# One pair of heads per step, the last query rows of both heads in one tile, and high q doubled by transfers within SBUF

## The chip, the core and the metric

The kernel runs on one core of one Trainium2 chip. A core has TensorE (PE; its weight loads are listed as PEld), VectorE (DVE), ScalarE (ACT), GpSimd (POOL) and SyncE (SP), which here only issues DMAs. They share SBUF (128 partitions), PE writes into PSUM, and 16 DMA engines move data. The time is the device's, in microseconds (us), and lower is better.

## The reference

Three stages run one after the other; the change is in the first alone.

```python
# attention, 4 x 8 heads, S = 576, D = 64
scores = q @ k.T / 8                     # per head
bias   = -(cum[:, None] - cum[None, :])  # cum = cumsum(max(s, 0))
scores = where(causal, -1e9, scores + minimum(bias, 0))
attn   = exp(scores - rowmax); attn /= attn.sum(-1) + 1e-9
x      = attn @ v                        # heads side by side: 576 x 512 per batch
# then: gated MLP with a product over tokens (moe), then 8 experts, one per token (moe2)
```

## The kernel before, in words

A program is written out per engine; engines meet only at semaphores, and each runs its instructions in the order in which they are written. 32 heads make 16 pairs. A head has 576 query rows: four tiles of 128 and a last one of 64 (`rows_of`); tile i needs the keys up to 128(i+1).

The precision scheme: q and k are split into a high and a low part. `q1` holds high q in a head's own 64 partitions and low q in the other 64, `k1` holds high k in both halves, `k2` low k beside four rows of the bias ("aug"), `q2` high q beside its four rows. So a tile of scores is two matmuls (`q1`·`k1`, L786, and `q2`·`k2`, L788) and one that adds the causal mask (L793). The second place of high q and of high k is filled by GpSimd's copies (`twice`, L484 and L487 for the main 512 columns, L476 and L477 for the last 64).

The loop runs over single heads, t = 0 to 33 (L862 on PE). Step t makes the scores of head t, DVE takes the row maxima (`row_max`, L661), ACT the exponentials with their sums (`exps`, L551), and PE turns the probabilities of head t-1 in four groups (`turn_probs`, L806) through the two banks of `tbank`; DVE (L667) and ACT (L558) copy each group out. The five tiles of scores share four banks of `sbank`: the last tile takes the place of tiles 0 and 1. In every second step the pair's k and q are turned (L748, L765, L755) through `obank`, the sums are inverted, widened on GpSimd (L495) and turned (L812), and the product with v of a finished pair (`attend`, L837, two parts) is written to `obank` and scaled by DVE into `xT` (L688).

SyncE issues, per pair, four DMAs of the bias rows (L398, L399), eight for k and q (L391 with 128 KB, L393 with 16 KB) and four for v (L405, L407), each group behind one semaphore wait. Ahead of the loop it issues the first loads, stores the bias rows to DRAM and reads them back (L420 to L399), and loads the MLP's weights (L425, L426). All of these go to one DMA queue. GpSimd splits the MLP's weights in 16 shares beside the loop (`weights`).

Of the kernel before, what the change touches and what calls it, by code (L numbers as in the profile page):

```python
# [13 lines left out]
P = 128  # L14
# [3 lines left out]
def moe_block(nc, q, k, v, s, w_in, g_ln, w_sg, b_sg, w_out, w_gate, w_local, w1, w2, out):  # L18
# [21 lines left out]
    PT_COLS = sum((i + 1) * w for i, w in enumerate([P] * FULL + [LAST]))  # L40
# [9 lines left out]
    aug_dram = nc.dram_tensor("aug_dram", (HEADS, 2, 4, S), F32).ap()  # L50
# [3 lines left out]
    with stack:  # L54
# [3 lines left out]
        def tensors(scope):  # L58
# [58 lines left out]
        recip_wide = ab("recip_wide", [P, ST, 2, D], F32)  # L117
        recipT = ab("recipT", [P, S], F32)
        probs = [ab(f"probs{u}", [P, OFF_P[-1] + SP], F32) for u in range(2)]
        k_raw = [ab(f"k_raw{u}", [P, ST, 2, D], F32) for u in range(2)]  # L120
        q_raw = [ab(f"q_raw{u}", [P, ST, 2, D], F32) for u in range(2)]
# [5 lines left out]
        nmax = [ab(f"nmax{u}", [P, ST], F32) for u in range(2)]  # L127
        sums = [ab(f"sums{u}", [P, 2, ST], F32) for u in range(2)]
        sums_eps = ab("sums_eps", [P, 2, ST], F32)
        recip = ab("recip", [P, 2, ST], F32)  # L130
# [101 lines left out]
        late_pads = sem("late_pads")  # L232
# [9 lines left out]
        aug_in = [sem(f"aug_in{c}") for c in range(4)]  # L242
        v_in = [sem(f"v_in{u}") for u in range(2)]
        kq_turned = sem("kq_turned")
        kq_high = sem("kq_high")
        kq_low = sem("kq_low")
        kq_twice = sem("kq_twice")
        scored = sem("scored")
        maxed = sem("maxed")
        exped = sem("exped")  # L250
        p_turned = sem("p_turned")
        p_left = [sem(f"p_left{n}") for n in range(4)]
# [3 lines left out]
        recip_turned = sem("recip_turned")  # L256
        recip_main = sem("recip_main")
# [65 lines left out]
        MAIN, TAIL = slice(0, FULL * P), slice(FULL * P, S)  # L323
        SHARES = 16
        FIRST_SHARE = 4
        own_rows = [slice(0, D), slice(D, P)]
        other_rows = [slice(D, P), slice(0, D)]
        wide_of = [sbank[:, 2 * i:2 * i + 2, :].rearrange("p a n -> p (a n)") for i in range(2)]

        GROUPS_OF = [[(0, 0), (0, 1), (0, 2)],  # L330
                     [(1, 1), (1, 2), (2, 2)],
                     [(0, 3), (0, 4), (1, 3), (1, 4)],
                     [(2, 3), (2, 4), (3, 3), (3, 4), (4, 4)]]
        GROUP_COLS = [sum(rows_of[i] for _, i in g) for g in GROUPS_OF]
        GROUP_AT = [sum(GROUP_COLS[:n]) for n in range(4)]
        ROWS = [slice(0, 3 * P), slice(3 * P, S)]
        R_TAIL = slice(3 * P, 3 * P + LAST)
        K_TAIL, Q_TAIL = slice(0, LAST), slice(LAST, 2 * LAST)

        def score_view(i, rows):  # L340
            if i < FULL:
                return sbank[0:rows, i, 0:W_P[i]]
            return sbank[0:rows, 0:2, 0:HALF]

        def probs_view(u, i, rows):
            w = probs[u][0:rows, OFF_P[i]:OFF_P[i] + W_P[i]]
            return w if i < FULL else w.rearrange("p (a n) -> p a n", a=2)
# [12 lines left out]
        def sets_of(p):  # L360
            return [2 * (p % 2), 2 * (p % 2) + 1]

        def k_pair(t):

            return (t + 3) // 2 if t % 2 and (t + 3) // 2 < PAIRS else None

        def q_pair(t):

            return t // 2 + 1 if t % 2 == 0 and t // 2 + 1 < PAIRS else None

        def inverted_pair(t):

            return t // 2 - 1 if t % 2 == 0 and t >= 2 else None

        def attended_pair(t):

            return t // 2 - 1 if t % 2 and t >= 3 else None

# [6 lines left out]
        def _(sp):  # L385
            def load_kq(p):
                b = p % 2
                for u in range(2):
                    for raw, src in ((k_raw, kf), (q_raw, qf)):
                        x = src[2 * p + u, :, :]  # L390
                        sp.dma_start(raw[b][:, 0:FULL, u, :],  # L391
                                     x[0:FULL * P, :].rearrange("(t p) d -> p t d", p=P)).then_inc(kq_in[b], 16)
                        sp.dma_start(raw[b][0:LAST, FULL, u, :], x[FULL * P:S, :]).then_inc(kq_in[b], 16)  # L393

            def load_aug(h):
                c = h % 4
                r = 0 if h % 2 else D
                sp.dma_start(k2[c][r:r + 4, :].bitcast(F32), aug_dram[h, 0, :, :]).then_inc(aug_in[c], 16)  # L398
                sp.dma_start(q2[c][r:r + 4, 0:S].bitcast(F32), aug_dram[h, 1, :, :]).then_inc(aug_in[c], 16)  # L399

            def load_v(p):
                b = p % 2
                for u in range(2):
                    x = vf[2 * p + u, :, :]
                    sp.dma_start(v_raw[b][:, 0:FULL, u, :],  # L405
                                 x[0:FULL * P, :].rearrange("(t p) d -> p t d", p=P)).then_inc(v_in[b], 16)
                    sp.dma_start(v_raw[b][0:LAST, FULL, u, :], x[FULL * P:S, :]).then_inc(v_in[b], 16)  # L407
# [12 lines left out]
            sp.dma_start(aug_dram, aug[:, :, :, :]).then_inc(aug_stored, 16)  # L420
            sp.wait_ge(aug_stored, 16)
            sp.wait_ge(consts, 2)
            load_aug(0)
            load_aug(1)
            sp.dma_start(win_raw[:, :, :], w_in.rearrange("(k p) n -> p k n", p=P)).then_inc(w_in_landed, 16)  # L425
            sp.dma_start(wout_raw[:, :, :], w_out.rearrange("(k p) n -> p k n", p=P)).then_inc(w_out_landed, 16)  # L426
            sp.wait_ge(late_sets, 6)
            load_aug(2)
            load_aug(3)
            load_v(0)  # L430
            load_v(1)
            for t in range(2, HEADS):
                if t + 2 < HEADS:
                    sp.wait_ge(scored, ST * (t - 1))
                    load_aug(t + 2)
                m = t // 2
                if t % 2 == 0 and m + 1 < PAIRS:
                    sp.wait_ge(kq_turned, 3 * m)
                    load_kq(m + 1)
                if t % 2 == 0 and m >= 2:  # L440
                    sp.wait_ge(av_done[1], m - 1)
                    load_v(m)

        @block.gpsimd
        def _(pool):
# [12 lines left out]
            pool.wait_ge(pool_own, 6)  # L458
            for u in range(2):
                nc.gpsimd.memset(v_raw[u][:, FULL, :, :], 0.0)  # L460
                nc.gpsimd.memset(q1[2 + u][:, S:SP].bitcast(F32), 0.0).then_inc(late_sets, 1)
            for u in range(2):
                pool.wait_ge(late_sets, 2 + u)
                nc.gpsimd.memset(k2[2 + u][other_rows[u], :].bitcast(F32), 0.0)
                nc.gpsimd.memset(q2[2 + u][other_rows[u], :].bitcast(F32), 0.0).then_inc(late_sets, 1)
            pool.wait_ge(late_sets, 4)
            for u in range(2):
                nc.gpsimd.memset(q2[2 + u][own_rows[u], S:SP].bitcast(F32), 0.0).then_inc(late_sets, 1)
                pool.wait_ge(late_sets, 5 + u)

            def twice(p, n):

                if n == 4:
                    pool.wait_ge(kq_high, 5 * p + 5)
                    for u, c in enumerate(sets_of(p)):
                        nc.gpsimd.tensor_copy(k1[c][other_rows[u], TAIL], k1[c][own_rows[u], TAIL].bitcast(F32))  # L476
# [14 lines left out]
            def widen(m):  # L491
                pool.wait_ge(inverted, m + 1)
                if m:
                    pool.wait_ge(recip_turned, m)
# [1311 lines left out]
```

## Time and profile before

| what | value |
|---|---|
| median of 3 runs | 879.79 us (879.1 to 881.36) |
| the profiled execution | 881.97 us, span 880.2 us |
| busy over the span | PE 775.4 us (88%), DVE 486.0, ACT 378.7, POOL 163.6 |
| chain that ended last | PE 82%, DVE 10%, ACT 3% |
| attention's scores begin, xT is whole | 28.06 us, 283.7 us |

The profile is of one execution. A busy PE row counts a matmul from its start to a modelled end, so neighbours overlap; where the pace matters, the distance between starts is read. "Idle before" is what an engine waited ahead of a group, and the name behind the arrow is what released it.

### The profile page before, as it was taken

Reading aid. Unit: us, or ns where it says so; the run is one execution under the profiler, and the core shown is the slowest. Engines: PE = TensorE matmul, PEld = TensorE weight load, DVE = VectorE, ACT = ScalarE, POOL = GpSimd, SP = SyncE. Lnnn points to the kernel's source line nnn. Section 1 sums busy time; section 2 is a strip of 40 time slices with the busy share of each in tenths; the row PEclk is TensorE's granted clock in tenths of the full one; section 3 lists DMA queues with packets and bytes.
Section 4 is the critical chain, followed back from the end, with each engine's and each line's share of the span. In section 5 each row is a group of like instructions: output and inputs, shape, how many; then the busy total and the mean of one; then the engine's idle time right before and its main releaser. Section 6 shows DMA issues by size and latency. Waiting matters only on the chain.

```text
span 880.2 us, 15547 instructions
## 1 busy us (share of the span) xinstructions
PE 775.4 (88%) x4885; PEld 649.7 (74%) x4886; DVE 486.0 (55%) x947; ACT 378.7 (43%) x846; POOL 163.6 (19%) x341
## 2 busy tenths in 40 slices
PE   2778888788888999999999997579999999999993
PEld 2566667566676899989899895458888888887772
DVE  8577777877775363453462353854644663726221
ACT  2576676766765340431431512334442551533110
POOL 4134454532222100000000000021122122221121
PEclk9999999999999999999999998579999999999997
DMA  6622232222210000010010012961543561611110
GB/s 156 192 57 57 58 71 54 54 64 57 64 26 23 3 1 1 1 54 0 0 54 0 0 55 71 365 239 38 222 164 119 206 235 49 225 32 34 41 42 16
DMA packets 81405, 70.41 MB, mean 80 GB/s; under 512 B 61960, under 2 KB 61960, under 8 KB 81322
## 3 DMA queue, kind: packets, MB, share of 16 engines
q1 hardware_dynamic: 77354, 58.49, 21.6%
q0 software_dynamic: 4000, 11.28, 3.9%
q8 instruction: 27, 0.44, 0.2%
q14 instruction: 24, 0.20, 0.1%
HBM read 59.72 MB, written 11.86 MB: 81 GB/s over the span
## 4 chain that ended last, share of the span: by engine, by line
PE 82%; DVE 10%; ACT 3%; issue 2%; DMA 1%; SPq 0%; POOL 0%; POOLq 0%; ACTq 0%; DVEq 0%
PE sbank L1091 25%; PE sbank L1684 10%; PE sbank L1686 9%; PE sbank L1685 9%; PE obank L837 5%; PE tbank L806 5%; PE sbank L786 4%; DVE nmax L661 3%; PE sbank L788 3%; PE obank L1139 2%; ACT probs L551 1%; DVE q L653 1%; PE tbank L1669 1%; PE tbank L1709 1%; PE sbank L793 1%
## 5 line engine op out<-in xcount | busy, mean ns | idle before, releaser
L551 ACT ACTIVATE probs<-sbank,nmax 128x128 f32<-128x128 f32 (+4 forms) x160 | 90.6, 568 | 62.3 <-DVE nmax L661 60.8
L806 PE MATMUL tbank<-ident,probs 128*128 128x128 f32 x480 | 75.7, 279 | 20.5 <-ACT pT L558 20.1
L786 PE MATMUL sbank<-k,q 128*128 128x256 f32 (+2 forms) x192 | 74.4, 393 | 16.3 <-ACT probs L551 14.7
L661 DVE TENSOR_REDUCE nmax<-sbank 128x1 f32<-128x128 f32 (+4 forms) x160 | 80.1, 532 | 7.5 <-PE sbank L793 5.9
L1684 PE MATMUL sbank<-w_high,xsT_h 128*128 x184 | 75.0, 407 | 1.9 <-DVE xsT_l L1609 1.7
L1193 DVE TENSOR_TENSOR w_low<-w_low,w_high (+1 forms) x64 | 74.0, 1218 | 0.7 <-ACT w_high L1549 0.3
L1686 PE MATMUL sbank<-w_low,xsT_h 128*128 x184 | 72.7, 395 | 0.0
L1685 PE MATMUL sbank<-w_high,xsT_l 128*128 x184 | 72.5, 394 | 0.0
L1684 PE MATMUL sbank<-w_high,hidT_h 128*128 x176 | 71.0, 403 | 0.1
L806 PEld LDWEIGHTS tbank<-ident,probs 128*128 128x128 f32 x480 | 51.1, 141 | 25.7 <-ACT pT L558 23.9
L1549 ACT CAST w_high<-w_low (+1 forms) x64 | 62.3, 1053 | 17.5 <-SPq L1438 17.5
L1686 PE MATMUL sbank<-w_low,hidT_h 128*128 x176 | 68.9, 391 | 0.0
L1685 PE MATMUL sbank<-w_high,hidT_l 128*128 x176 | 68.8, 391 | 0.0
L1480 POOL DMA_INDIRECT out_dram<-y,sid x25 | 25.3, 1011 | 217.8 <-DVE y L1645 214.4
L1469 POOL COPY gid<-slots 128x1 int32 (+1 forms) x25 | 6.4, 255 | 290.1 <-DVE slots L1369 281.5
L788 PE MATMUL sbank<-k,q 128*128 128x256 f32 (+2 forms) x192 | 60.3, 319 | 0.0
L786 PEld LDWEIGHTS sbank<-k,q 128*128 128x128 f32 x192 | 37.9, 197 | 23.5 <-ACT probs L551 18.3
L1572 ACT CAST hidT_h<-tbank 128x512 fp32r<-128x512 f32 x22 | 12.9, 586 | 92.8 <-PE tbank L1709 92.8
L1645 DVE TENSOR_SCALAR y<-sbank,sid 128x512 f32<-128x512 f32 x22 | 16.5, 751 | 64.1 <-PE sbank L1686 63.3
L837 PE MATMUL obank<-pT,v_raw 128*64 128x192 f32 (+4 forms) x512 | 50.2, 339 | 0.3 <-ACT recipT L562 0.3
L1091 PE MATMUL sbank<-wsg_h,vn_h 128*128 128x288 f32 x160 | 48.3, 302 | 2.2 <-DVE vn_l L1025 1.9
L1091 PE MATMUL sbank<-wsg_l,vn_h 128*128 128x288 f32 x160 | 47.9, 299 | 0.0
(246 smaller groups left out, 1939.7 us busy)
## 6 DMA issues: line engine op xcount, KB each, us to landing
w_low<-in_moe_w_dram SPq DMA_DIRECT2D x16, 2048.0 KB, 14.1
k_raw<-in_k_dram SPq DMA_DIRECT2D x32, 128.0 KB, 2.3
q_raw<-in_q_dram SPq DMA_DIRECT2D x32, 128.0 KB, 2.4
v_raw<-in_v_dram SPq DMA_DIRECT2D x32, 128.0 KB, 2.3
x_dram<-x SPq DMA_DIRECT2D x4, 1024.0 KB, 4.4
win_raw<-in_moe_w_in_dram SPq DMA_DIRECT2D x1, 2048.0 KB, 7.9
wsg_raw<-in_moe_w_sg_dram SPq DMA_DIRECT2D x1, 1152.0 KB, 5.8
wout_raw<-in_moe_w_out_dram SPq DMA_DIRECT2D x1, 1024.0 KB, 10.8
```

The lines of the kernel that those rows point to most:

```text
L551: nc.scalar.activation(probs_view(u, i, r), score_view(i, r), ACT.Exp, bias=nmax[u][0:r, i:i + 1], accum_out=sums[(t // 2) % 2][0:r, u, i: ...
L661: nc.vector.tensor_reduce(nmax[u][0:r, i:i + 1], score_view(i, r), ax, ALU.max, negate=True).then_inc(maxed, 1)
L786: nc.tensor.matmul(dst, q1[c][:, q_cols], k1[c][:, cols], start=True, stop=False)
L788: nc.tensor.matmul(dst, q2[c][:, q_cols], k2[c][:, cols], start=False, stop=last)
L806: mm = nc.tensor.transpose(tbank[:, n % 2, at:at + P], probs[h % 2][:, OFF_P[i] + P * j:OFF_P[i] + P * (j + 1)], ident[:, :])
L837: mm = nc.tensor.matmul(obank[own_rows[u], c, lo:lo + w], v_raw[m % 2][:, j, u, :], pT[(2 * m + u) % 3][:, at:at + w], start=(j == 0), sto ...
L1091: mm = nc.tensor.matmul(dst, a[:, i, lhs_cols], b[:, i, rhs_cols], start=(n == 0), stop=(n == 3 * len(pairs) - 1))
L1193: nc.vector.tensor_sub(w, w.bitcast(F32), piece(w_high, high_place, i).bitcast(F32)).then_inc(wlow_done, 1)
L1549: nc.scalar.copy(piece(w_high, high_place, i), piece(w_low, low_place, i).bitcast(F32)).then_inc(whigh_done, 1)
L1684: nc.tensor.matmul(dst, xh, wh, start=first, stop=False)
L1685: nc.tensor.matmul(dst, xl, wh, start=False, stop=False)
L1686: return nc.tensor.matmul(dst, xh, wl, start=False, stop=last)
```

## The change

Attention alone is rewritten; all that stands behind it is the same code.

- The loop runs over pairs, g = 0 to 18. In step g PE turns q and k of pair g, makes all scores of pair g-1 but tile 3 of its second head, finishes pair g-2 (that tile, the rest of the turned probabilities, the second part of the product with v, the sums) and makes the first part of the product with v of pair g-3.
- The last 64 query rows of both heads stand in one 128-row tile: `q1` and `q2` of the second head hold their columns shifted by 64 with zeros beside them, so that four pairs of matmuls add up in two banks (`last_scores`); one maximum and one exponential serve both heads, and its four key blocks are turned into one bank and kept in `pT4`. The second part of the product with v has separate matmuls for these 64 columns.
- k, q and their last rows are copied out of PSUM in one instruction of 128 partitions (before: one per head), high q into the new tile `q_both`. Four transfers within SBUF per pair, 64 x 576 fp32 each (147 KB), bring it from there into `q1` and `q2` of both heads (`double_q`). GpSimd copies k only.
- SyncE's loads of the last rows of two heads are one DMA; its order per pair is bias rows, `double_q`, k and q of the next pair, the last bias row, v.

```diff
@@ SyncE
+            def load_aug(m):
+                c, b = sets(m), m % 2
+                sp.dma_start(k2[c + 1][AUG_ROWS[1], :].bitcast(F32), aug_k_dram[2 * m + 1, :, :]).then_inc(aug_in[b], 16)
+                for u in range(2):
+                    sp.dma_start(q2[c + u][AUG_ROWS[u], Q_ALL[u]].bitcast(F32),
+                                 aug_q_dram[2 * m + u, :, BOTH_ALL[u]]).then_inc(aug_in[b], 16)
+            def double_q(m):
+                sp.wait_ge(tails_high, m + 1)
+                for u in range(2):
+                    for t in (q1, q2):
+                        sp.dma_start(t[sets(m) + u][OWN[u], Q_ALL[u]].bitcast(F32),
+                                     q_flat[OWN[u], BOTH_ALL[u]].bitcast(F32)).then_inc(q_doubled[m % 2], 16)
...
-            for t in range(2, HEADS):
-                if t + 2 < HEADS:
-                    sp.wait_ge(scored, ST * (t - 1))
-                    load_aug(t + 2)
...
+            for m in range(1, PAIRS):
+                if m >= 2:
+                    sp.wait_ge(scored[1][3], m - 1)
+                load_aug(m)
+                double_q(m)
+                if m + 1 < PAIRS and m >= 1:
+                    sp.wait_ge(k_turned, m)
+                    load_kq(m + 1)
+                sp.wait_ge(k2_copied, m + 1)
+                load_aug_k(m)
+                if m >= 2:
+                    sp.wait_ge(av_done[0], m - 1)
+                load_v(m)
@@ ScalarE: q leaves PSUM once the copies of the pair before have read q_both
+            def split_q(m):
+                act.wait_ge(q_turned, m + 1)
+                if m:
+                    act.wait_ge(q_doubled[(m - 1) % 2], 64 * turn_of(m - 1))
+                nc.scalar.mul(q_flat[:, BOTH_MAIN], obank[:, 1, :], SCALE).then_inc(q_high, 1)
@@ TensorE
+            def last_scores(m):
+                for a in range(2):
+                    for u in range(2):
+                        score(sbank[:, a, 0:HALF], sets(m) + u, Q_LAST[u], slice(a * HALF, (a + 1) * HALF),
+                              u == 0, u == 1 and a == 0)
+                nc.tensor.matmul(sbank[:, 1, HALF - LAST:HALF], ident_bf[:, :], mask_last[:, :], start=False,
+                                 stop=True).then_inc(last_scored, 1)
...
+            for g in range(PAIRS + 3):
+                a, b, c = g - 1, g - 2, g - 3
+                if alive(g):
+                    turn_q(g)
+                if alive(b):
+                    pe.wait_ge(exped[0][3], b + 1)
+                    scores(1, 3, b)
+                if alive(c):
+                    pe.wait_ge(recip_main, c + 1)
+                    pe.wait_ge(left[1][0], c + 1)
+                    attend(c, 0)
...
+                if alive(a):
+                    pe.wait_ge(q_doubled[a % 2], 64 * turn_of(a))
+                    pe.wait_ge(k1_copied, 3 * a + 3)
+                    pe.wait_ge(aug_in[a % 2], 48 * turn_of(a))
+                    pe.wait_ge(aug_k_in[a % 2], 16 * turn_of(a))
+                    scores(0, 0, a)
+                    scores(0, 1, a)
```

On PE, in the middle of the stage, the rows from one pair's first part of the product with v to the next tiles of scores. Before (`pT` is a turned probability tile, `probs` one not yet turned, `k1_1` the set 1 of `k1`):

```order
L806 MATMUL tbank<-ident,probs0 128x128 x2
L837 MATMUL obank<-pT0,v_raw1 64x384 [waits recip_main,v_in1,recip_tail,p_left1,p_left0]
L837 MATMUL obank<-pT1,v_raw1 64x384
L837 MATMUL obank<-pT0,v_raw1 64x256
L837 MATMUL obank<-pT1,v_raw1 64x256
L837 MATMUL obank<-pT0,v_raw1 64x128
L837 MATMUL obank<-pT1,v_raw1 64x128
L786 MATMUL sbank<-k1_1,q1_1 128x384
```

And now:

```order
L763 MATMUL obank<-ident,q_raw0 128x128 [waits x_left1,kq_in0]
L763 MATMUL obank<-ident,q_raw0 128x128 x3
L792 MATMUL sbank<-k1_1,q1_1 128x512 [waits exped03]
L793 MATMUL sbank<-k2_1,q2_1 128x512
L800 MATMUL sbank<-mask_bf,ident_bf 128x128
L839 MATMUL obank<-pT0,v_raw1 64x384 [waits left10,recip_main]
L839 MATMUL obank<-pT1,v_raw1 64x384
L839 MATMUL obank<-pT0,v_raw1 64x256
L839 MATMUL obank<-pT1,v_raw1 64x256
L839 MATMUL obank<-pT0,v_raw1 64x128
L839 MATMUL obank<-pT1,v_raw1 64x128
```

The turning of q with its wait for the loads (`kq_in0`) now stands ahead of the product, three instruction groups apart, at the head of the step.

On SP, one pair of the loop before:

```order
L398 DMA k2_0<-aug_dram 4x576 [waits scored]
L399 DMA q2_0<-aug_dram 4x576
L391 DMA k_raw0<-in_k_dram 128x4x64 [waits kq_turned]
L393 DMA k_raw0<-in_k_dram 64x64
...
L391 DMA q_raw0<-in_q_dram 128x4x64
L393 DMA q_raw0<-in_q_dram 64x64
L405 DMA v_raw1<-in_v_dram 128x4x64 [waits av_done1]
L407 DMA v_raw1<-in_v_dram 64x64
```

And one pair now, from v on:

```order
L415 DMA v_raw<-in_v_dram 128x4x64 [waits av_done0]
L415 DMA v_raw<-in_v_dram 128x4x64
L417 DMA v_raw<-in_v_dram 64x2x64
L422 DMA k_1<-aug_k_dram 4x576 [waits scored13]
L424 DMA q_0<-aug_q_dram 4x576
L424 DMA q_1<-aug_q_dram 4x576
L435 DMA q_0<-q_both 64x576 [waits tails_high]
L435 DMA q_0<-q_both 64x576
L435 DMA q_1<-q_both 64x576 x2
L405 DMA k_raw<-in_k_dram 128x4x64 [waits k_turned]
```

Between v, which waits for the first part of the product, and the next k and q there now stand seven DMAs, four of them the copies within SBUF.

## Rows read from the trace of the kernel before

**Rows 1.** Windows: stretch, length, busy PE, PEld, DVE, ACT, POOL; PEclk, DMA share, GB/s.

```profile
0.00:28.00 28.00, 10.03 (x39) 7.10 (x40) 21.06 (x42) 8.65 (x17) 9.82 (x30) 1.00 0.75 202
28.00:283.80 255.80, 217.05 (x1762) 170.13 (x1762) 185.40 (x423) 173.10 (x519) 92.46 (x219) 1.00 0.25 57
283.80:880.20 596.40, 548.34 (x3084) 472.51 (x3084) 279.59 (x483) 196.93 (x311) 61.28 (x93) 0.95 0.24 84
...
204.28:220.20 15.92, 13.46 (x111) 10.59 (x111) 11.91 (x28) 11.03 (x35) 4.08 (x9) 1.00 0.26 59
```

**Rows 2.** Waits of PE in one pair, 188.36 to 204.28.

```profile
PE tbank L806 <- ACT pT L558: 1.4, 1, 1.4
PE sbank L786 <- ACT probs L551: 1.0, 1, 1.0
```

**Rows 3.** Timeline of PE in one pair: start, length, what.

```profile
209.69 1.52 PE L837 MATMUL obank<-pT,v_raw 128*64 128x384 f32 x12
211.14 0.45 PE L786 MATMUL sbank<-k,q 128*128 128x384 f32 x1
...
211.64 0.47 PE L786 MATMUL sbank<-k,q 128*128 128x512 f32 x1
...
212.26 0.50 PE L806 MATMUL tbank<-ident,probs 128*128 128x128 f32 x3
...
213.13 0.20 PE L793 MATMUL sbank<-mask_bf,ident_bf 128*128 128x64 bf16 x1
213.26 1.64 PE L837 MATMUL obank<-pT,v_raw 128*64 128x192 f32 x20
214.82 0.66 PE L806 MATMUL tbank<-ident,probs 128*128 128x128 f32 x4
215.32 0.60 PE L748 MATMUL obank<-ident,k_raw 128*128 128x128 f32 x4
215.76 0.71 PE L806 MATMUL tbank<-ident,probs 128*128 128x128 f32 x5
```

**Rows 4.** Timeline of SP's issues, one pair: start, length, what.

```profile
205.87 0.40 SPq L391 DMA_DIRECT2D k_raw<-in_k_dram  x1
...
206.87 0.59 SPq L391 DMA_DIRECT2D q_raw<-in_q_dram  x1
...
214.94 0.38 SPq L405 DMA_DIRECT2D v_raw<-in_v_dram  x1
215.35 0.52 SPq L407 DMA_DIRECT2D v_raw<-in_v_dram  x1
...
217.10 0.49 SPq L398 DMA_DIRECT2D k<-aug_dram  x1
217.63 0.29 SPq L399 DMA_DIRECT2D q<-aug_dram  x1
```

**Rows 5.** DMA issues of the whole run: KB each, median us from issue to landing.

```profile
q_raw<-in_q_dram SPq DMA_DIRECT2D x32, 16.0 KB, 2.1
```

**Rows 6.** Groups by line and form, 100 to 275: count, busy, mean ns, idle before.

```profile
L551 ACT ACTIVATE probs<-sbank,nmax 64x576 f32<-64x576 f32 x23 | 17.0, 740 | 0.0
L533 ACT CAST k<-obank 64x512 fp32r<-64x512 f32 x20 | 11.6, 580 | 0.2
```

**Rows 7.** Timeline and window of the start.

```profile
6.56 0.52 SPq L413 DMA_DIRECT2D wsg_raw<-in_moe_w_sg_dram  x1
14.07 0.50 SPq L420 DMA_DIRECT2D aug_dram<-aug  x1
18.45 0.31 SPq L398 DMA_DIRECT2D k<-aug_dram  x1
19.77 0.40 SPq L425 DMA_DIRECT2D win_raw<-in_moe_w_in_dram  x1
28.06 0.58 PE L786 MATMUL sbank<-k,q 128*128 128x256 f32 x1 [1.50 <-DVE wsg_l L701]
19.77:31.10 11.33, 9.04 (x37) 6.07 (x35) 6.12 (x11) 5.24 (x12) 1.66 (x4) 1.00 0.94 307
```

More of the change, by code:

```diff
@@ L39, in moe_block @@
     OFF_P = [sum(W_P[:i]) for i in range(ST)]
-    PT_COLS = sum((i + 1) * w for i, w in enumerate([P] * FULL + [LAST]))
+    PT_COLS = sum((i + 1) * P for i in range(FULL)) + P
     qf = q.rearrange("b h s d -> (b h) s d")
@@ L126, in moe_block @@
         q2 = [ab(f"q2_{c}", [P, SP], F32R) for c in range(4)]
[L127 to L130, printed above, removed]
+        q_both = ab("q_both", [P, ST * 2, D], F32R)
+        nmax = ab("nmax", [P, 2 * FULL + 1], F32)
+        sums = ab("sums", [P, 2 * FULL + 1], F32)
+        sums_eps = ab("sums_eps", [P, 2 * FULL + 1], F32)
+        recip = ab("recip", [P, 2 * FULL + 1], F32)
         heads.close()
@@ new lines, in split_k, with exps @@
+            def split_k(m):
+                act.wait_ge(k_turned, m + 1)
+                nc.scalar.copy(k1[sets(m)][:, MAIN], obank[:, 0, :]).then_inc(k_high, 1)
+            def exps(u, i, m):
+                n = u * FULL + i
+                act.wait_ge(maxed[u][i], m + 1)
+                nc.scalar.activation(probs[u][:, OFF_P[i]:OFF_P[i] + W_P[i]], sbank[:, i, 0:W_P[i]], ACT.Exp,
+                                     bias=nmax[:, n:n + 1], accum_out=sums[:, n:n + 1]).then_inc(exped[u][i], 1)
@@ new lines, in last_exps, with probs_out @@
+            def last_exps(m):
+                n = 2 * FULL
+                act.wait_ge(last_maxed, m + 1)
+                nc.scalar.activation(probs4[:, 0:S].rearrange("p (a n) -> p a n", a=2), sbank[:, 0:2, 0:HALF], ACT.Exp,
+                                     bias=nmax[:, n:n + 1], accum_out=sums[:, n:n + 1]).then_inc(last_exped, 1)
+            def probs_out(u, n, m):
+                w = P * len(GROUPS_OF[n]) + (P if (u, n) == (1, 1) else 0)
+                act.wait_ge(turned[u][n], m + 1)
+                nc.scalar.copy(pT[(2 * m + u) % 3][:, GROUP_AT[n]:GROUP_AT[n] + w],
+                               tbank[:, n % 2, 0:w]).then_inc(left[u][n], 1)
@@ new lines, in turn_last_probs, with turn_recips, turn_recip_tail @@
+            def turn_last_probs(m):
+                for j in range(FULL):
+                    mm = turn(tbank[:, 1, P * j:P * (j + 1)], probs4[:, P * j:P * (j + 1)])
+                mm.then_inc(last_turned, 1)
+            def turn_recips(m):
+                for i in range(FULL):
+                    mm = turn(obank[:, 0, P * i:P * (i + 1)], flat(recip_wide[:, i, :, :]))
+                mm.then_inc(recip_turned, 1)
+            def turn_recip_tail(m):
+                nc.tensor.matmul(tbank[:, 1, 0:LAST], recip_last[:, :], fold[:, :], start=True,
+                                 stop=True).then_inc(recip_tail_turned, 1)
```

808 lines of the change are left out of this document (383 added, 425 removed).

## The prediction

> **What bounds the kernel now.** I read the windows by stage first, then PE's waits, then the timeline of one pair, and SP's issues last, because the change gives SP a new part. The windows [rows 1] show three stretches: 28.0 us until the first scores, 255.8 us of attention, 596.4 us of the rest, whose code is untouched. The profiled execution took 881.97 us, 1.77 more than its span of 880.2; the median of the three runs shown is 879.79, so the profile lies 2.2 above it. My sum starts from 881.97.
>
> One pair takes 15.92 us, and the reader is to see there that no engine is full: PE is busy for 13.46 (a busy sum that overlaps), DVE 11.91, ACT 11.03, POOL 4.08, DMA a quarter. The list of waits [rows 2] says where PE's missing time is: 1.4 us ahead of the last group of probabilities, whose bank ACT has yet to empty, and 1.0 us ahead of the last tile of scores, whose banks ACT's exponentials hold. So PE occupies 15.92 - 2.4 = 13.5 us per pair, and the rest is latency round trips between PE, DVE and ACT within one head. 16 pairs of it make the 255.8.
>
> **The change: the work of a pair on PE.** All by distances between starts [rows 3].
> - Transposes: 30 of probabilities, 5 of sums and 10 of k and q become 25, 4 and 9. Four start within 215.76 - 215.32 = 0.44 us, 0.11 each, so 7 fewer are worth -0.77.
> - Scores: the last tile was 2 heads x 4 matmuls of 288 columns; now it is 8 of the same in one tile. Nothing changes but one mask matmul less, 213.26 - 213.13 = 0.13.
> - The last 64 sums take one small matmul in place of a transpose: +0.15 at most.
> - Product with v: the first part is as before, 211.14 - 209.69 = 1.45. The second part keeps its columns (1664 over both heads) but has 18 matmuls where it had 10, each shown as two records. Before it takes 214.82 - 213.26 = 1.56. If columns set the pace it stays 1.56. If each record costs the mean 1.56/20 = 0.078, 36 take 2.8. I take 2.05 (+0.5): 0.11 each for the 64- and 128-column ones, the pace of the transposes, the nearest row with short matmuls.
>
> Sum: 13.5 - 0.77 - 0.13 + 0.15 + 0.5 = 13.25 us per pair if PE never waits; between 12.75 and 14.0 by the two ends of the last item.
>
> **ACT, DVE and POOL.** ACT loses one exponential of 0.74, two of the four copies of k and q at 0.58 [rows 6], the copy of the sums (to DVE) and two small tails, and gains one copy of a bank: 11.0 - 0.74 - 1.16 - 0.57 - 0.44 + 0.5 = 8.6. DVE loses a maximum, one subtraction of k and two copies of groups, and takes over the sums: about 10.3. POOL stays below half. None of them reaches 13. I also laid one step out in time from the order and these durations: with three pairs in flight beside the one whose q and k are turned, every wait in PE's step is met 0.5 to 3 us before PE comes to it (the nearest are the copy ahead of the third group of the second head, and low q ahead of the tails). So I cost both of today's waits, 2.4 us, as gone; what is late next is not on these engines.
>
> **SP is late next.** k and q of the next pair are now loaded behind v, the bias rows and the four copies, and PE's step begins with turning q, which waits for that load. Round the loop, from the start of a step: turning q 0.44, one tile of 512 columns 0.62 (212.26 - 211.64), first part of the product with its tail 1.52 [rows 3], sum 2.58; then SP wakes (0.04) and issues v at 0.41, 0.63 and 0.56, bias rows at 0.53 and twice 0.33, four copies, and k and q, four of 128 KB at 0.63 and the first of the two small ones at 0.56; the last lands 2.1 after its issue [rows 4, 5]. (An issue takes its length plus 0.04.) A copy of 64 x 576 has its nearest row in the 64 x 576 piece of w_sg, 0.52 + 0.04 [rows 7], so 2.2 for four; the bounds are 4 x 0.33 = 1.3 (a bias row) and 4 x 0.63 = 2.5. Sum: 2.58 + 0.04 + 1.60 + 1.19 + 2.24 + 3.08 + 2.1 = 12.8 us, from 11.9 to 13.1. That is just under PE's 13.25. The two nearly coincide, so I take 13.3 a pair, where the old one was 15.92.
>
> The data of the copies: 0.59 MB per pair. The saturated stretch [rows 7] moved 307 GB/s at a share of 0.94, so they need 1.9 us of the engines, and the pair's DMA share goes from 0.26 of 15.9 (4.1 us) to 6.0 of 13.3 us: 0.45. That much is hidden; q_both is wanted again only at the next step's start, some 5 us after the last issue of a copy.
>
> Here a rule of the Trainium skill speaks against the change. The queue moves 57 to 307 GB/s in the windows [rows 1, 7], but no row times a large transfer on 64 partitions by itself. "SBUF — State Buffer", section "Door 1: The DMA port swizzle", says that 64 adjacent partitions use half the ports, measured at 196 GB/s. By it the copies take 3.0 us instead of 1.9, an estimate from that page; issued over 2.2 us, they would push k and q back by 0.8 us, the round to 13.6 and the time by 12 x 0.3 to 848, inside the range; my sum does not use it.
>
> **The ends of the stage.** Before, the bias rows go to DRAM at 14.07, the read-back starts at 18.45, the MLP's weights are issued at 19.77 and the scores start at 28.06 [rows 7]. SP now has four fewer issues ahead of 14.07 (2.2 us), so the bias rows leave at 12; three stores instead of one, back at 17.5. Then 3 bias rows, 4 copies, one row and v, 5.4 us: the weights are issued at 23 and the queue is full for the same 11.3 us, to 34.4. The scores of pair 0 start at about 24, but the copies of pair 1 and k and q of pair 2 (1.18 MB, 3.8 us) stand behind the weights in the same queue: step 2 starts at 38.8. Step 2 has no product yet (11.8 us); steps 3 to 14 take 12 x 13.3 = 159.6; 15 waits for no load, 13.2; 16 turns no q and k, 12.2. Step 17 finishes pair 15: about 6.7 us of PE and 1.5 of round trips, 8.2; then its first part of the product and the last scaling, 2.9. End: 38.8 + 11.8 + 159.6 + 13.2 + 12.2 + 8.2 + 2.9 = 246.7, where it was 283.8. That is -37.1; 881.97 - 37.1 = 844.9. By the median it would be 842.7. I forecast 844.
>
> **The rivals.**
> 1. The short matmuls cost less and the issue of a copy is cheap: PE 12.75 and SP 11.9 per pair, so about 12.8, and k and q of pair 2 come through beside the weights (38.8 becomes 35). 844 - 14 x 0.5 - 3.8 = 833. For it: columns, not instructions, set PE's pace in the long pieces. Against: the transposes of 128 columns pay 0.11.
> 2. Copies lengthen SP's round: k and q really wait for all the copied bytes, or the records cost 0.078 each: 14.1 a pair, 844 + 14 x 0.8 = 855. For it: one queue for all, in order.
> 3. New round trips: a step laid out by hand hides no jitter, and DVE's last copy ends less than 1 us ahead of the next step's first maximum. If PE waits 1.6 us per pair again, 14.9: 844 + 14 x 1.6 = 866.
> 4. Slower than before. The copies within SBUF read and write the same partitions while everything else goes through the same queue. If they run at 90 GB/s or less, 0.59 MB take 6.6 us or more and k and q, another 2.6 us of the engines, land only behind them: from a start of copies at 5.4 that is 5.4 + 1.5 + 6.6 + 2.6 + 0.5 = 16.6 a pair, 844 + 14 x 3.3 = 890. It decides from about 16 us a pair, a rate of 100 GB/s. Against: the loads of 256-byte pieces alone run at 60 GB/s with a share of 0.26, some 230 if full, and the copied pieces are 2304 bytes long.
> 5. The change moves nothing, because the stage is bound elsewhere: PE's 13.5 of 15.92 and no other engine over 12 speak against; only 2.4 us would be to be had if the fold saved nothing, and that alone is worth 30.
>
> **How the numbers follow.** Forecast 0.56, rival 1 0.16, rival 2 0.13, rival 3 0.08, rival 4 0.05, rival 5 0.02. The forecast's own range is 837 to 851 (0.5 us a pair). With rivals 1 and 2 the range is 828 to 862; outside lie rivals 3 to 5 and the far tail of rival 1. What this kernel's measurement can tell from no change is about 0.3%, 2.6 us. Faster: forecast, rivals 1 to 3, 0.93; within 0.3%: 0.02; slower: 0.05.
>
> **What would show it.** A pair's period of 13.3 in the middle of the stage. Among PE's waits, the two of 1.4 and 1.0 are gone; what remains stands at the turning of q and is ended by a DMA, below 0.5 us. PE busy per pair within 0.3 of 13. SP's copies are issued 0.5 to 0.6 apart and are done before the next q leaves PSUM, so ACT's split of q never waits for them. DMA share 0.4 to 0.5. xT is whole at 247, and the rest takes 596 again. The forecast is wrong in its mechanism if PE waits more than 1 us per pair, for ACT or DVE (rival 3) or for the loads (rivals 2 and 4), or if the rest of the kernel changes its length.

## The result, and the profile after

The changed kernel takes 858.05 us (median of 4 runs, 855.16 to 858.86) where the kernel before took 880.58 on the same chip (4 runs, 879.1 to 881.59): a ratio of 0.974, interval 0.971 to 0.9769. It is faster, inside the range of 828 to 862, and 14 us slower than the forecast of 844: 22.5 us came where 37 were forecast. The profiled execution took 858.82 us, with a span of 857.1; the sum in the prediction ended at 844.9.

The windows of the kernel after, by stage, then one undisturbed step, then two short stretches of it. The columns are those of [rows 1].

```profile
28.00:261.40 233.40, 204.66 (x1910) 166.26 (x1909) 154.88 (x354) 140.30 (x421) 89.41 (x197) 0.96 0.45 106
261.40:857.10 595.70, 547.61 (x3084) 471.39 (x3084) 279.77 (x483) 197.05 (x311) 60.61 (x88) 0.95 0.24 84
125.50:138.80 13.30, 12.38 (x121) 10.18 (x121) 9.95 (x23) 8.95 (x27) 7.36 (x16) 1.00 0.50 115
121.00:124.00 3.00, 3.00 (x42) 2.77 (x39) 1.61 (x4) 2.32 (x8) 2.75 (x5) 1.00 0.96 217
131.00:137.27 6.27, 6.27 (x76) 5.60 (x75) 4.65 (x14) 4.73 (x16) 3.02 (x6) 1.00 0.77 176
```

The attention ends at 261.4 instead of 283.8, and the rest takes 595.7 where it took 596.4: all of the gain lies in the attention. The granted clock of that stretch is 0.96, where it was 1.00. A pair has gone from 15.92 us to 13.30 here, and the DMA's share over a pair from 0.26 to 0.50. While copies and the next k and q are under way it is 0.77 to 0.96, at only 176 to 217 GB/s; the start had needed 307 GB/s for 0.94 [rows 7].

PE's waits over the attention (microseconds in total, times, the longest):

```profile
PE obank L763 <- DMA k_raw<-in_q_dram: 26.0, 14, 8.2
PE obank L839 <- DVE recipT L702: 0.8, 1, 0.8
PE sbank L792 <- ACT probs L571: 0.7, 1, 0.7
```

Both waits of [rows 2] are gone. In their place stands one at the turning of q, for the last piece of the loads. From the start of step 3 to the start of step 15 (56 to 228) it is 17.8 us in 13 waits, 1.37 us each:

```profile
PE obank L763 <- DMA k_raw<-in_q_dram: 17.8, 13, 2.4
```

The chain of waits through one step (start, length, what) shows why:

```profile
123.33 2.15 DMA k_raw<-in_q_dram
125.47 0.04 issue
125.52 0.66 PE obank L763 x4
126.17 0.23 PE sbank L792
126.41 0.24 PE sbank L793
126.64 0.07 PE sbank L800
126.71 1.47 PE obank L839 x12
128.20 0.37 SPq L415
...
129.17 0.61 SPq L417
...
131.02 0.51 SPq L435
...
133.59 0.59 SPq L405
...
135.94 0.65 SPq L409
136.63 2.15 DMA k_raw<-in_q_dram
...
138.82 0.66 PE obank L763 x4
```

This is the round through SyncE that the prediction walked: turn q, first part of the product (2.68 us until SP issues again), then 16 issues from v (L415) to the last of k and q (L409) with 0.04 us between them, the last of which starts 8.43 us after the first; then 2.15 us to the landing. ACT, DVE and POOL are not on it.

The steps (distance between starts of turning q) are not all alike, though: 13.22 and 13.30 us where nothing disturbs them, but 14.23 as the mean of steps 3 to 14. Three rows of PE's timeline, with the wait in brackets:

```profile
42.88 1.11 PE L763 MATMUL obank<-ident,q_raw 128*128 128x128 f32 x4 [8.20 <-DMA k_raw<-in_q_dram]
56.24 0.66 PE L763 MATMUL obank<-ident,q_raw 128*128 128x128 f32 x4 [0.33 <-DMA k_raw<-in_q_dram]
153.61 1.12 PE L763 MATMUL obank<-ident,q_raw 128*128 128x128 f32 x4 [2.41 <-DMA k_raw<-in_q_dram]
```

In the steps from 2 on, four transposes take 1.1 us behind the waits of 8.20 and 2.41 us and 0.66 otherwise. The windows behind these two waits and behind one of 1.75 name the reason:

```profile
42.88:46.00 3.12, 3.12 (x13) 2.60 (x14) 0.95 (x2) 1.57 (x4) 0.00 (x0) 0.50 0.45 103
153.60:157.00 3.40, 3.39 (x13) 1.98 (x15) 1.22 (x2) 1.85 (x4) 0.48 (x2) 0.51 0.00 0
84.06:86.50 2.44, 2.44 (x11) 1.32 (x13) 1.17 (x2) 1.74 (x4) 1.15 (x2) 0.74 0.00 0
```

The granted clock is at its lower level there, 1.2 GHz (0.50 and 0.51), or partly so (0.74), after PE had waited 8.20, 2.41 and 1.75 us. (Not always: the wait of 2.09 us ahead of 213.27 was followed by a step at 1.00.) What it costs is read from a whole step at a lower clock and one at 1.00:

```profile
84.06:98.73 14.67, 14.01 (x122) 11.01 (x122) 10.01 (x23) 8.95 (x27) 6.34 (x13) 0.88 0.45 104
125.52:138.82 13.30, 12.38 (x121) 10.18 (x122) 9.95 (x23) 8.95 (x27) 7.36 (x16) 1.00 0.50 115
```

PE is busy for 14.01 us instead of 12.38. Three of the steps 3 to 14 are such (14.01, 13.89 and 13.95 us busy), together 4.7 us. And the wait of 2.41 has its own cause in SP's issues of the step before:

```profile
144.33 2.44 SPq L435 DMA_DIRECT2D q<-q_both  x4
146.81 2.12 SPq L405 DMA_DIRECT2D k_raw<-in_k_dram  x1
148.97 0.51 SPq L405 DMA_DIRECT2D q_raw<-in_q_dram  x1
```

One issue takes 2.12 us where its like takes 0.59. Seven such single issues (1.02 to 2.12) stand in steps 3 to 14: one of v, one copy, and five loads of k and q right behind the copies. Together they are 6.3 us longer than their likes. The DMA packets in the trace show what else moves in these moments. One queue on the page is of the kind "instruction" (packets, MB, share over the whole run):

```profile
q8 instruction: 28, 0.46, 0.2%
```

Its packets, 16 KB each and 0.9 to 1.6 us long, come once in 13 to 17 us in these steps, and each of the seven long issues runs at the same time as one of them (146.81 to 148.93 beside a packet from 146.98 to 148.55). Beside the other five packets no issue is longer than its like by over 0.3 us.

### The profile page after: what moved, and what is told of

It reads as the page before. It is cut to its first block, busy times and chain, and to the rows that moved or that the text cites. A ratio compares the mean times of both kernels' runs of the same rounds, so it can differ in the third digit from the quotient of the medians.

```text
span 857.1 us, 15546 instructions
## 1 busy us (share of the span) xinstructions
PE 766.4 (89%) x5045; PEld 647.2 (76%) x5046; DVE 454.8 (53%) x877; ACT 345.2 (40%) x750; POOL 155.6 (18%) x307
## 4 chain that ended last, share of the span: by engine, by line
PE 73%; SPq 15%; DMA 5%; issue 3%; DVE 2%; ACT 1%; POOL 0%; POOLq 0%; ACTq 0%; DVEq 0%
PE sbank L1129 26%; PE sbank L1722 10%; PE sbank L1724 10%; PE sbank L1723 10%; SPq L405 5%; SPq L435 4%; DMA k_raw<-in_q_dram 4%; PE obank L839 3%; PE obank L1177 2%; SPq L409 2%; PE obank L763 2%; PE tbank L1707 1%; PE tbank L1747 1%; SPq L415 1%; PE obank L1747 1%
## 5 line engine op out<-in xcount | busy, mean ns | idle before, releaser
L675 DVE TENSOR_REDUCE nmax<-sbank 128x1 f32<-128x128 f32 (+3 forms) x128 | 57.2, 481 | 43.3 <-PE sbank L800 42.9
L792 PE MATMUL sbank<-k,q 128*128 128x256 f32 (+1 forms) x192 | 73.7, 392 | 1.7 <-DMA k<-aug_k_dram 1.0
L571 ACT ACTIVATE probs<-sbank,nmax 128x128 f32<-128x128 f32 (+3 forms) x128 | 67.2, 536 | 11.7 <-DVE nmax L675 11.6
L793 PE MATMUL sbank<-k,q 128*128 128x256 f32 (+1 forms) x192 | 60.8, 324 | 0.0
L763 PE MATMUL tbank<-ident,probs 128*128 128x128 f32 x400 | 59.8, 282 | 0.5 <-DVE pT L687 0.3
L502 POOL CAST k<-k 64x576 fp32r<-64x576 f32 x64 | 42.5, 664 | 72.3 <-DVE k L670 69.4
L763 PEld LDWEIGHTS tbank<-ident,probs 128*128 128x128 f32 x400 | 45.6, 145 | 4.0 <-issue 2.9
L1129 PE MATMUL sbank<-wsg_h,vn_l 128*128 128x288 f32 x160 | 47.1, 294 | 0.0
```

Of the source, the lines that this page charges most:

```text
L571: nc.scalar.activation(probs[u][:, OFF_P[i]:OFF_P[i] + W_P[i]], sbank[:, i, 0:W_P[i]], ACT.Exp, bias=nmax[:, n:n + 1], accum_out=sums[:, n ...
L675: nc.vector.tensor_reduce(nmax[:, n:n + 1], sbank[:, i, 0:W_P[i]], AX_X, ALU.max, negate=True).then_inc(maxed[u][i], 1)
L763: return nc.tensor.transpose(dst, src, ident[:, :])
L792: nc.tensor.matmul(dst, q1[c][:, q_cols], k1[c][:, k_cols], start=first, stop=False)
L793: return nc.tensor.matmul(dst, q2[c][:, q_cols], k2[c][:, k_cols], start=False, stop=last)
L1129: mm = nc.tensor.matmul(dst, a[:, i, lhs_cols], b[:, i, rhs_cols], start=(n == 0), stop=(n == 3 * len(pairs) - 1))
```

## The experiments

All were timed in 3 to 5 rounds beside the kernel before (medians 881.76, 882.71 and 882.14 in the three jobs). "After" is the changed kernel, to which every edit is made.

### Taking k and q out from behind the copies

```diff
@@ e1: k and q of a pair are loaded a step earlier
+            sp.wait_ge(k_turned, 1)
+            load_kq(2)
...
-                if m + 1 < PAIRS and m >= 1:
-                    sp.wait_ge(k_turned, m)
-                    load_kq(m + 1)
+                if m + 2 < PAIRS:
+                    sp.wait_ge(k_turned, m + 1)
+                    load_kq(m + 2)
```

> SyncE issues k and q of pair m+2 behind the copies of pair m (once pair m's k has left its buffer), so they have a whole step to land. Nothing else changes. Theory (SyncE's round sets the step: product with v of pair m-2, v, bias rows, four copies, k and q, landing): the 13.2 to 15.5 us of a step fall to PE's own 12.3, the waits of 0.3 to 2.4 us for the loads at the turning of q vanish, and with them the stretches at 0.87 to 0.90 of the clock; k and q of pair 2 also pass ahead of the MLP's weights. 858 - 12 x 1.9 - 2 to 5 = 830 to 834. Rival (the queue's bytes, 0.45 to 0.5 of the DMA engines, are the limit): the wait moves to the copies or the bias rows and the time stays within 3 of 858.

Measured: 835.24 us (834.85 to 836.89), ratio 0.9481 (0.9464 to 0.9497), 23 us faster than after with the same instructions. That is 1 us above the expected 834, and far from the rival's 858. Every step from step 3 on takes 12.19 to 12.20 us at clock 1.00, and no wait stands at turning q. So the wait for k and q was the whole excess of the steps, and PE's own step is 12.2, not the 13.25 of my sum. One step was lost elsewhere: step 2 takes 19.90 us, with PE held for 7.0 us by probabilities. ACT makes them only behind its split of q, which waits 7.2 us for the copies of the pair before (L557 <- DMA q_both). Nearly saturated DMAs fill that gap, the MLP's weights with the copies behind them:

```profile
36.54:44.18 7.64, 0.61 (x7) 0.37 (x6) 1.41 (x3) 1.38 (x4) 0.00 (x0) 0.82 0.98 245
60.00:200.00 140.00, 140.00 (x1402) 116.12 (x1401) 113.70 (x265) 103.29 (x314) 72.04 (x147) 1.00 0.55 126
```

In the second row PE is busy for all 140 us; the same stretch of after has 125.94.

### GpSimd instead of the queue

```diff
@@ e4: SyncE's four copies go, GpSimd makes them
-                double_q(m)
...
+                    pool.wait_ge(tails_high, m + 1)
+                    for u in range(2):
+                        for t in (q1, q2):
+                            nc.gpsimd.tensor_copy(t[sets(m) + u][OWN[u], Q_ALL[u]],
+                                                  q_flat[OWN[u], BOTH_ALL[u]].bitcast(F32)).then_inc(q_doubled[m % 2], 16)
```

> The four copies of high q are GpSimd's (four of 64 x 576, some 0.66 us each) and no transfer: all else stays. Theory (four copies stand in SyncE's round): round 13.2 - 2.4 = 10.8, below PE's 12.3, so steps of 12.3, no wait for the loads, and 858 - 12 x 1.9 = 835, with step 2 somewhat earlier, too. Rival (the transfers relieve GpSimd or VectorE): GpSimd's 3.7 to 8.6 us a step grow by 2.7, k of the next pair is late, steps of 14 or more, 858 or slower.

Measured: 825.55 us (825.11 to 826.25), ratio 0.9368 (0.9353 to 0.9384). From step 3 on all steps take 12.19 to 12.20 us, and the DMA share falls again:

```profile
60.00:200.00 140.00, 140.00 (x1381) 115.80 (x1381) 114.94 (x268) 103.05 (x311) 98.26 (x188) 1.00 0.34 76
```

GpSimd's busy time over the kernel rises from 155.6 to 196.3 us and delays nobody. The start gains too: step 2 begins at 35.19 instead of 42.88, since no copies stand in the queue there. The expected 835 counted only the steps at 1.9 us each; the start's 7.7 us lie beside that. So the copies on the queue cost 32.5 us against the same four copies on GpSimd.

Single long issues do not need the copies. Six of them (1.25 to 1.91 us) stand in steps 3 to 14 here too, with no copy on the queue and a DMA share of 0.34, and again each beside a packet of q8; the round has room for them:

```profile
126.03 1.89 SPq L405 DMA_DIRECT2D q_raw<-in_q_dram  x1
```

### What in the copies costs: issues, bytes, or the half of the partitions

Four edits change only `double_q` and what counts or prepares its copies. Three of them leave out part of the sum of scores: e6 brings half of the columns of high q (zeros stand for the rest), e7 leaves out high q in `q2`, and e8 brings no high q into `q1` and `q2` at all. The instructions of PE and ACT stay the same.

```diff
@@ e3: two transfers of twice the size, q1 and q2 side by side in one tile q12
-                    for t in (q1, q2):
-                        sp.dma_start(t[sets(m) + u][OWN[u], Q_ALL[u]].bitcast(F32),
-                                     q_flat[OWN[u], BOTH_ALL[u]].bitcast(F32)).then_inc(q_doubled[m % 2], 16)
+                    sp.dma_start(q12[sets(m) + u][OWN[u], :, Q_ALL[u]].bitcast(F32),
+                                 q_flat[OWN[u], BOTH_ALL[u]].bitcast(F32).unsqueeze(1)
+                                 .to_broadcast([D, 2, S])).then_inc(q_doubled[m % 2], 16)
@@ e6: four transfers of half the columns
+                        x, y = Q_ALL[u].start, BOTH_ALL[u].start
+                        sp.dma_start(t[sets(m) + u][OWN[u], x:x + HALF].bitcast(F32),
+                                     q_flat[OWN[u], y:y + HALF].bitcast(F32)).then_inc(q_doubled[m % 2], 16)
@@ e7: two of the four
-                    for t in (q1, q2):
+                    for t in (q1,):
@@ e8: two transfers of 128 partitions and 536 columns into a tile that nobody reads
+                    sp.dma_start(q_aside[:, u, :].bitcast(F32),
+                                 q_flat[:, BOTH_ALL[u].start:BOTH_ALL[u].start + S - 40].bitcast(F32)).then_inc(q_doubled[m % 2], 16)
```

> The four copies of a pair become two, each from the same source into q1 and q2 of one head (laid side by side in one tile): the same bytes in half the issues. Theory (SyncE's issue time is in the round): 1.2 us less per round while PE needs 12.3, so steps of about 12.4 to 13.3 and 858 - 12 x 1.2 = 844. Rival (bytes, or a slow path of 64 partitions): the two land as late as the four, 856 to 860.

> Each of the four copies moves half of its columns (288 of 576), so half of high q is left out (zeros); issues and their number stay. Halving the issues alone had left the clean steps at 13.1 (13.2 before) because the loads of k and q behind them were issued more slowly. Theory (the bytes of the copies fill the queue ahead of k and q): k and q's issues stay at 0.5 to 0.6 and the waits of 0.8 to 2.4 us at the turning of q shrink, but four issues of 0.61 still stand in the round, so steps of 12.8 to 13.2 with fewer long ones: 850. Rival (issue time alone): 857, as with whole copies.

> Only q1 gets its copies, two of the four (q2's high q is left out, zeros): half the issues and half the bytes. Theory (issues and bytes both stand in the round, whichever is longer): the round loses 1.2 us, 13.2 - 1.2 = 12.0, below PE's 12.2; steps of 12.2 to 12.5 and 840. If the bytes alone or the issues alone did it, one of the kernels with half of one of them would be as fast.

> The four copies of 64 partitions (590 KB) become two of 128 partitions by 536 columns (549 KB) into a tile aside, so high q is left out of the scores: nearly the bytes of before, in two issues, but spread over all partitions. With the two merged transfers of 64 partitions the copies landed 4.2 us after their issue and the time was 853.2. Theory (a transfer on 64 partitions moves its bytes at about half the rate): they land after 3.0 us or less, k and q's issues stay at 0.5 to 0.6, steps of 12.2 to 12.6, 842. Rival (the bytes cost the same on any partitions): landing 4.0, 852.

| | issues | KB in all | partitions | landing of one copy | undisturbed step | mean of steps 3 to 14 | median, us | ratio |
|---|---|---|---|---|---|---|---|---|
| after | 4 | 576 | 64 | 2.5 | 13.22, 13.30 | 14.23 | 858.05 | 0.974 (0.971 to 0.9769) |
| e6 | 4 | 288 | 64 | 2.1 | 13.20 to 13.49 | 14.11 | 855.22 | 0.97 (0.9662 to 0.9737) |
| e3 | 2 | 576 | 64 | 4.2 | 13.07 to 13.18 | 13.88 | 853.16 | 0.9688 (0.966 to 0.9716) |
| e7 | 2 | 288 | 64 | 2.4 | 12.21 to 12.30 | 12.78 | 836.71 | 0.9479 (0.9451 to 0.9507) |
| e8 | 2 | 536 | 128 | 2.5 | 12.19 to 12.21 | 12.80 | 837.19 | 0.9493 (0.9465 to 0.9521) |

Against what was expected: e6's 855.22 lies by the rival's 857 and not at 850; e3's 853.16 lies at neither 844 nor 856 to 860; e7 (840) and e8 (842) came 3 and 5 us faster.

The landings are from the lists of DMA issues, of e3 and then of e8:

```profile
q<-q_both SPq DMA_DIRECT2D x32, 288.0 KB, 4.2
k_raw<-in_k_dram SPq DMA_DIRECT2D x32, 128.0 KB, 3.8
```
```profile
q_aside<-q_both SPq DMA_DIRECT2D x32, 268.0 KB, 2.5
k_raw<-in_k_dram SPq DMA_DIRECT2D x32, 128.0 KB, 2.7
```

Half the bytes with four issues (e6) changes little, in the undisturbed steps and in the mean: it is SP's issuing that sets the pace, and the bytes do not make the long steps either. Half the issues with all the bytes (e3) changes little as well, for another reason: the two issues take 1.28 us instead of 2.44, but k and q behind them are issued in 0.75, 1.33 and 0.67 us instead of 0.59, 0.57 and 0.50, and land in 3.8 instead of 2.6. Halving both (e7) brings PE's own 12.2 in undisturbed steps; with 12.78 in the mean it still waits for loads in most, 0.2 to 1.2 us, where e1 and e4 have 12.19. And e8 moves nearly e3's bytes with e3's number of issues, but over 128 partitions, and has e7's time. The same part of a step, 4 us from 1.15 us behind the start of the copies, in e3 and in e8:

```profile
115.50:119.50 4.00, 4.00 (x57) 3.56 (x56) 2.54 (x7) 3.31 (x11) 1.95 (x3) 1.00 0.99 219
```
```profile
120.82:124.82 4.00, 4.00 (x57) 3.56 (x56) 2.53 (x7) 3.33 (x11) 1.94 (x3) 1.00 0.96 269
```

The DMA engines are as good as full in both, but move 219 GB/s in e3 and 269 in e8. A transfer of 288 KB on 64 partitions takes 4.2 us, one of 268 KB on 128 partitions 2.5. e3 also reads each source row twice, which e8 does not; that e7 and after, with plain sources on 64 partitions, need 2.4 to 2.5 us for only 144 KB speaks for the partitions, but no run separates the two. The Trainium skill's "SBUF — State Buffer", section "Door 1: The DMA port swizzle", says that 64 adjacent partitions reach only half the ports; the 4.2 us against 2.5 agree with it.

### The weights at the start

```diff
@@ e2, e5: win_raw and wout_raw are issued behind the next v; e5 = e1 + e2
-            sp.dma_start(win_raw[:, :, :], w_in.rearrange("(k p) n -> p k n", p=P)).then_inc(w_in_landed, 16)
...
+                if m == 1:
+                    sp.dma_start(win_raw[:, :, :], w_in.rearrange("(k p) n -> p k n", p=P)).then_inc(w_in_landed, 16)
@@ e9 = e1 + the weights in KT pieces, one behind each of the first v
+                if m <= KT:
+                    k = m - 1
+                    sp.dma_start(win_raw[:, k, :], w_in[P * k:P * (k + 1), :]).then_inc(w_landed[k % 2], 16)
+                    sp.dma_start(wout_raw[:, k, :], w_out[P * k:P * (k + 1), :]).then_inc(w_landed[k % 2], 16)
```

> The MLP's weights (3 MB) are issued behind the loads of pair 2 and v of pair 1 in place of ahead of them. Theory (step 2 waits 8.2 us for k and q that stand behind the weights in one queue): step 2 starts at 34 to 35 in place of 42.9, and all of the stage moves by that: 850. Rival (the same bytes only collide later): k and q of pair 3 then wait behind the weights, step 3 is late by 6 to 8 us and the time is 856 to 860.

> Loads of k and q two pairs ahead, and the MLP's weights issued behind v of pair 1. With the loads ahead alone the time was 835.2, and its step 1 (from 35.5) took 19.9 us in place of 12.2, waiting for the copies and a bias row of pair 1 behind the weights. Theory (one queue in order: what stands behind 3 MB waits): now the weights stand behind these, only the copies of pair 2, wanted a step later, stand behind the weights; 5 to 7 us come back, 829. Rival (the weights cost their 11 us of a full queue wherever they stand, as when they were moved alone): a later step loses as much, 835.

> k and q two pairs ahead, and the MLP's weights in four pieces of 768 KB, one behind v of each of the pairs 1 to 4, in place of 3 MB at once. Wherever the 3 MB stood, one step took 19.6 to 19.9 us in place of 12.2. Theory (a full queue of 11 us ahead of the copies costs the step that waits for them; 2.8 us at a time fits into a step's slack): steps 1 to 5 all take 12.2 to 12.5, 835 - 7 = 828. Rival (the queue's total load in the first steps costs, however it is cut): 2 us in each of four steps, 835.

Each of the three came out nearest to one of its own two numbers: e2 just below its rival's 856 to 860, e5 at its rival's 835, e9 near its theory's 828. Measured: e2 855.88 us (854.79 to 860.34), ratio 0.9724 (0.9692 to 0.9756), the same as after within the intervals. Step 2 begins 8.3 us earlier, at 34.59, but then takes 18.05, and the next 15.66 behind a wait of 6.40. e5 takes 834.26 (832.99 to 835.21), ratio 0.9456 (0.9426 to 0.9485), with one step of 19.55: the same loss as e1, later. e9 takes 826.46 (824.36 to 826.87), ratio 0.9375 (0.9361 to 0.9389), with steps 1 and 2 of 13.26 and 11.47 and then 12.19 to 12.45. So with k and q loaded ahead 3 MB in one block cost the steps once, in both places tried, 8.4 us in step 2 (19.90 against 11.47) and 7.4 in step 3 (19.55 against 12.19), and in four pieces almost nothing.

### What the lower clock costs

```diff
@@ e10: four fp32 transposes of the identity, whose result is overwritten, ahead of turning q
+                if 3 <= g < PAIRS:
+                    pe.wait_ge(x_left[1], g - 2)
+                    for _ in range(4):
+                        nc.tensor.matmul(obank[:, 1, 0:P], ident[:, :], ident[:, :], start=True, stop=True)
```

> The changed kernel, and ahead of the turning of q four fp32 matmuls of 128 columns into the bank that it is about to overwrite (0.85 us of work where PE waits 0.8 to 2.4 us for the loads in nearly every step). Theory (the waits of about 2 us let TensorE's clock fall to 1.2 GHz, shown as 0.87 to 0.90 over a step, and each such step is 1 to 1.5 us longer): the low stretches in the steps become rare, the clean steps stay at 13.2, and the time falls by 2 to 4 us to 855. Rival (low stretches come by chance or cost nothing, since PE has 1 us to spare per step): 858, or up to 5 more if the added work stands on the path.

Measured: 849.76 us (5 runs, 848.5 to 852.58), ratio 0.9631 (0.9618 to 0.9644): more work, 8 us faster than after and 5 us faster than expected. From step 3 on, none has a clock below 1.00; undisturbed steps stay at 13.2 to 13.5. The windows behind a wait of 1.81 us and behind the next, of 0.89:

```profile
84.00:87.00 3.00, 3.00 (x25) 1.99 (x24) 1.94 (x3) 2.04 (x5) 0.00 (x0) 1.00 0.02 5
98.00:101.00 3.00, 2.99 (x23) 1.98 (x24) 1.69 (x3) 2.05 (x5) 1.04 (x2) 1.00 0.02 5
```

Steps 3 to 14 take 164.7 us in place of 170.75, 6.0 less. Not all of that is the clock: the three slow steps of after hold 4.7 us of it, and the long issues of e10 are fewer (five, 4.8 us over their likes, where after has 6.3), which the edit does not explain. Three long steps remain (15.16, 14.24 and 14.42), with long issues in them (2.21 and 1.88 us for a pair that usually takes 0.92, and a single one of 1.60): those do not come from PE's clock. That the filler holds the clock up is likely but rests on few cases: it leaves PE only one wait over 1.1 us in these steps, the one of 1.81, and other runs have waits as long with and without a fall behind them.

### Both cures together

e11 is e1 and e4, with the weights in pieces as in e9.

> High q doubled by GpSimd (825.6 alone), with k and q two pairs ahead and the weights in four pieces. With GpSimd's copies every step from 2 on was already PE's 12.19 us and only the first ones took longer (13.6 and 11.5 with 0.5 us of waiting for loads). Theory (nothing is left in SyncE's round): 0.5 to 1 us at most, 825. Rival (the loads of v, held for 1 to 2 us in steps 2 to 4 behind the weights, still cost something): 822.

Measured: 823.63 us (820.92 to 824.62), ratio 0.9337 (0.9316 to 0.9358), the lowest median of all, but the interval overlaps that of e4 (0.9353 to 0.9384), and neither 825 nor 822 is ruled out. From step 3 on the steps take 12.19 to 12.20 us, PE's own, so SP's queue has nothing left to give there.

## Why the prediction was right in its range, and what in its sum was not

- **The old waits go: right.** Both are gone, and the only one of any size is for the loads at turning q.
- **That wait below 0.5 us: wrong.** It is 1.37 us per step, and the prediction called itself wrong in its mechanism if PE waits more than 1 us per pair for the loads. By its own sign the step was misjudged: not PE and SP side by side, but SP alone, with PE idle for 1.1 us (13.3 - 12.2) even where nothing disturbs it.
- **SP is late next: right; its round of 12.8: short by 0.5.** The walk round the loop names the right pieces. Measured from 125.52 to 138.82 they are 2.68 (2.62 in the sum), v 1.62 (1.60), bias rows 1.20 (1.19), copies 2.57 (2.24), k and q 3.04 (3.08) and 2.15 and 0.04 to the landing and on (2.1). So 13.30, above the stated 11.9 to 13.1. That undisturbed steps hit the assumed 13.3 is luck: the 13.3 was taken from PE's 13.25, and that is wrong, too.
- **PE's own step of 13.25: wrong.** It is 12.2 (e1, e4; after's step 15, which waits for no load: 12.21). The second part of the product with v takes 1.85 us from its start to the next scores, so the 2.05 assumed for it was near; the scores, the transposes and what remained of today's round trips in my 13.5 must hold the rest, which I have not split. It cost the forecast nothing by itself, since SP's round is longer, but it hid that the queue is the bound: I priced PE and SP as coinciding, and the copies as nearly free. They cost 32.5 us (e4).
- **Steps 3 to 14 at 13.3 each, 159.6: the step that failed.** They took 170.75, 11.15 more. The sum put nothing there for delays, and with SP always the last, each delay of its round is passed on. Two kinds showed: seven single long issues, together 6.3 us above their likes; and three steps at a lower clock, 4.7. The two add up to 11.0, but they are not independent (a long issue makes the wait that the clock falls after), so the split is not exact.
- **Step 2 at 38.8, then 11.8: mis-sized.** It began at 42.88 (+4.1) and took 13.36 (+1.6), at clock 0.82. I let the queue drain at the rate of [rows 7] and put the pair's 1.18 MB behind it at the same rate; SP in fact stood in issues of 1.47, 3.46, 2.54 and 3.49 us until 40.65. Some 1 us of it varies from run to run: e10, whose start is the same code, begins step 2 at 41.76.
- **DMA's share 0.45: 0.50.** The bytes were priced at 307 GB/s; in the burst the queue is full at 217 (219 in e3). But half the bytes (e6) save only 2.8 us, within the intervals, and the last load lands 2.15 us after its issue where 2.1 was taken, so in after the slower copies cost next to nothing; they show in e3. The Trainium skill's "Door 1: The DMA port swizzle" ("SBUF — State Buffer"), which my sum did not use, agrees with the copies' speed (4.2 us on 64 partitions against 2.5 on 128). The 848 worked out from it was 4 us nearer, but by the wrong way: k and q were not pushed back by the copied bytes.
- **The ends: right within 2 us** (steps 15 and 16 1.9 shorter, the last part 0.2), and the rest of the kernel is unchanged.
- **The rivals.** Rival 2 (855, chance 0.13) came nearest in its number, 14.1 a pair against a mean of 14.23. Neither of its two causes is borne out in after: k and q land as fast with half of the copied bytes (2.6 and 2.5 us in both, e6), though they suffer in e3, and the records do not cost 0.078 each: 36 would take 2.8 us, and they take 1.60 (234.66 to 236.26). So the nearness is luck. Rival 1 was nearer on PE (12.75 for 12.2) but not on SP or the start. Rivals 3, 4 and 5 fell: from 28 us on no wait for ACT or DVE of over 0.8 us, and the queue with the copies moves 217 GB/s, far above 90.

Open: why single issues take 1 to 2 us. The copies are not the reason, since e4 has six without them. Two kinds are to be told apart. At a full queue issues lengthen by themselves (1.3 us in every step of e3 at a share of 0.99, 1.5 to 3.5 behind the 3 MB). The single ones in after all coincide with a packet of q8, the instruction queue, and so do those of e1, e2, e4, e6, e7, e8 and e11 in these steps; in e9 and e10 all but one do. That the fetch of instructions holds the issue up is what this suggests, but no run changed the fetches, so it is not shown. With k and q loaded two pairs ahead, or the copies off the queue, the long issues no longer matter.

## What to carry to other kernels

A queue that serves in order is an engine of its own: add up its issues between the event that wakes it and the load that PE waits for, and when that sum equals the step, either load one step further ahead (e1: 23 us for no work) or take instructions off the queue (e4: 32.5 us). A forecast that rests on two nearly equal bounds should add what their jitter costs, here 0.9 us per step of 13.3, because the critical round has no cover. A copy within SBUF is not free because the DMA's mean share is low: here its issues cost first (four in place of two, e6 against e7: 18.5 us), its bytes only where they filled the queue ahead of the awaited load (e3). Look at the share in that burst, and prefer all partitions over half of them (e8).

## What was not expected of the hardware

- Waits of 1.75 to 2.4 us once per step were followed by stretches of 2.4 to 3.4 us at a granted clock of 0.51 to 0.74 (at 84.06, 153.60 and 183.27); waits of 1.57 and 2.09 were not, nor one of 2.20 in e2, so the length of the wait alone does not decide. With filler ahead of the wait (four transposes, 1.1 us) the clock stayed at 1.00 from step 3 on and the kernel was 8 us faster (e10).
- An issue on SP usually takes 0.3 to 0.65 us whatever its size (four copies: 2.44 us at 576 KB, 2.43 at 288 KB), so for small transfers the count of DMAs on the round is the price.
- On 64 partitions a transfer within SBUF took 4.2 us for 288 KB, on 128 partitions 2.5 us for 268 KB.
- With 3 MB in the queue ahead, single issues took up to 3.6 us (e1), so everything that SP has still to issue is late too.
- All seven single issues of 1.02 to 2.12 us in steps 3 to 14 of after, and all six of 1.25 to 1.91 in e4, ran beside a 16 KB packet of the instruction queue q8.
